# Attention inputs with a place each, V sums on two engines, softmax sums from a column of ones, logits by token

## The reference

```python
# q, k, v: [2, 8, 768, 64]; block, window = 32, 16
k_sum = k.reshape(B, H, nb, block, D).max(axis=3)
v_sum = v.reshape(B, H, nb, block, D).mean(axis=3)
scores_l = scale * q @ k.T, masked to |i - j| < window
scores_s = scale * q @ k_sum.T + log(block)
a = exp(concat(scores_l, scores_s) - max)
a = a / (sum(a) + 1e-09)
x = a @ concat(v, v_sum)                       # -> [1536, 512]
logits1 = x @ w_gate;  noise_scale = log1p(exp(x @ w_noise))
x1 = top-2 mixture of 8 experts (512 -> 1024 -> 512) of x
logits2 = x1 @ w_gate2;  skip = x1 @ w_skip
out = x1 + gate * chosen expert(x1) where skip > 0
```

## Time and profile before

| | us |
|---|---|
| median of 3 runs (lowest, highest) | 775.97 (775.58, 776.98) |
| the profiled execution's own time | 778.27 |
| its span, first to last instruction | 776.4 |
| PE busy (share of the span) | 667.5 (86%) |
| DVE / ACT / POOL busy | 378.0 / 322.7 / 201.1 |
| mean granted clock of PE | 0.948 |

### The profile page before, as it was taken

One profiled execution on the slowest core, in us unless ns is written; L12 is line 12 of the kernel. 1 busy time (PEld: TensorE's weight loads), 2 busy tenths in 40 slices (PEclk: granted clock), 3 DMA queues, 4 the chain that ended last, 5 costly groups with the idle time before them and its releaser, 6 DMA issues.

```text
span 776.4 us, 13848 instructions
## 1 busy us (share of the span) xinstructions
PE 667.5 (86%) x3906; PEld 534.9 (69%) x3906; DVE 378.0 (49%) x664; ACT 322.7 (42%) x613; POOL 201.1 (26%) x254
## 2 busy tenths in 40 slices
PE   4685876659999999999999999977569997999894
PEld 3464654448787887878878787855448776778673
DVE  3392685935453625434344345431636756556621
ACT  2272786025353524435244244422115656455511
POOL 1537330712222222232222222220221221222221
PEclk9996999779999999999999999997779999999998
DMA  9994795324555545635446264645326657667211
GB/s 204 193 210 134 205 279 188 129 82 135 149 160 150 151 94 138 161 70 156 117 118 183 48 176 125 173 118 182 148 82 189 191 173 261 205 196 230 55 39 16
DMA packets 91199, 116.67 MB, mean 150 GB/s; under 512 B 52500, under 2 KB 52500, under 8 KB 91088
## 3 DMA queue, kind: packets, MB, share of 16 engines
q1 hardware_dynamic: 81584, 94.75, 41.2%
q0 software_dynamic: 9568, 21.37, 14.7%
HBM read 99.72 MB, written 20.71 MB: 155 GB/s over the span
## 4 chain that ended last, share of the span: by engine, by line
PE 77%; DVE 6%; DMA 5%; issue 3%; POOL 3%; SPq 2%; ACT 2%; POOLq 0%; ACTq 0%; DVEq 0%
PE bank L690 60%; PE bank L706 5%; PE bank L616 3%; PE bank L665 3%; SPq L425 2%; DVE col_val L1168 2%; POOL stage L922 2%; DMA stage<-in_moe_w 2%; DMA stage<-in_v 1%; PE bank L605 1%; PE bank L577 1%; PE bank L767 1%; PE bank L588 1%; ACT pt_sb L800 1%; DVE w_lo L1077 1%
## 5 line engine op out<-in xcount | busy, mean ns | idle before, releaser
L1077 DVE TENSOR_TENSOR w_lo<-stage,w_hi (+1 forms) x128 | 152.0, 1221 | 29.6 <-ACT w_hi L807 27.5
L690 PE MATMUL bank<-w_hi,xt_hi 128*128 128x512 f32 x336 | 139.7, 416 | 16.3 <-DVE w_lo L1077 7.9
L1224 DVE TENSOR_TENSOR ht_lo<-bank,ht_hi 128x512 fp32r<-128x512 f32 x84 | 58.1, 691 | 185.2 <-ACT ht_hi L879 185.2
L807 ACT CAST w_hi<-stage (+1 forms) x128 | 129.1, 1049 | 28.2 <-PEq L732 23.6
L690 PE MATMUL bank<-w_hi,ht_hi 128*128 128x512 f32 x336 | 138.6, 412 | 0.0
L690 PE MATMUL bank<-w_lo,xt_hi 128*128 128x512 f32 x336 | 134.6, 401 | 0.0
L690 PE MATMUL bank<-w_lo,ht_hi 128*128 128x512 f32 x336 | 131.4, 391 | 0.0
L876 ACT ACTIVATE h_sb<-bank 128x512 f32<-128x512 f32 x84 | 50.3, 598 | 112.8 <-PE bank L690 112.8
L690 PE MATMUL bank<-w_hi,xt_lo 128*128 128x512 f32 x336 | 93.1, 400 | 0.0
L879 ACT CAST ht_hi<-bank 128x512 fp32r<-128x512 f32 x84 | 49.2, 586 | 100.9 <-PE bank L706 100.9
L690 PE MATMUL bank<-w_hi,ht_lo 128*128 128x512 f32 x336 | 91.1, 392 | 0.0
(11 more groups left out here) (111 smaller groups left out, 732.2 us busy)
## 6 DMA issues: line engine op xcount, KB each, us to landing
stage<-in_moe_w SPq DMA_DIRECT2D x128, 512.0 KB, 4.3
v_win<-in_v SPq DMA_DIRECT2D x24, 192.0 KB, 4.8
x_moe<-zeros SPq DMA_DIRECT2D x13, 256.0 KB, 4.3
stage<-in_k SPq DMA_DIRECT2D x16, 192.0 KB, 4.6
stage<-in_q SPq DMA_DIRECT2D x16, 192.0 KB, 4.4
stage<-in_v SPq DMA_DIRECT2D x16, 192.0 KB, 4.4
x_att<-x_sb SPq DMA_DIRECT2D x12, 256.0 KB, 4.1
x_sb<-x_moe SPq DMA_DIRECT2D x12, 256.0 KB, 2.8
```

The lines of the kernel that those rows point to most:

```text
L690: last = eng.matmul(ps[:], *every[i], start=(i == 0), stop=(i == len(every) - 1))
L807: eng.copy(piece(w_hi[n % SETS], j), stage[:, j, :]).then_inc(s_hi, 1)
L1077: eng.tensor_tensor(piece(w_lo[n % SETS], j), stage[:, j, :], piece(w_hi[n % SETS], j).bitcast(F32), ALU.subtract)\
L1224: eng.tensor_tensor(ht_lo[:, half].rearrange("p k n -> p (k n)"), ps_ht[half][:], ht_hi[:, half].bitcast(F32).rearrange("p k n -> p (k n)" ...
```

## The change

1. Places. K and Q of batch 0 and half of its V lie side by side in `stage`; the other half, and all of batch 1, in `late_raw`, which lies where the first expert's rounded weights (`w_hi0`, `w_lo0`) are written later. No load of K, Q or V waits any more. K and Q come by pairs of token tiles for all heads (256 KB a DMA), V by pairs of heads (384 KB a DMA). The constants are split: the identity first, the rest after the first Q.
2. Order. Q is turned two tiles at a time, when its tiles need it (steps 3 and 5); batch 1 follows in steps 6 to 12, V of batch 1 in step 13.
3. V is summed for heads 0 to 3 on POOL as before, for heads 4 to 7 by one reduction on DVE (line 1032 of the changed kernel).
4. `v_win` has a 65th column of ones for each head; the product with V gives the row sums in PSUM, `normalise` reads them there, and the exponentials have no accumulator. A head takes 74 columns in two joined banks.
5. Logits by token: the turned x is the stationary operand and `wgate` the moving one, straight into `ps_gate`. The copy on ACT and the transpose back are gone in both routers.
6. The first expert's pieces are loaded in tiles 2 to 5; the 13 blocks of zeros follow after the last store of x.

```diff
@@ -315,32 +329,30 @@
         STEPS = NG * NT
         TURN_LAG, PV_LAG = 2, 3
         NORM_LAG = NG - 1 + PV_LAG
-        X_LAG, GATE_LAG = NORM_LAG + 1, NORM_LAG + 2
-        LAST = STEPS - NG + GATE_LAG + 1
+        X_LAG, GATE_LAG = NORM_LAG + 1, NORM_LAG + 3
+        LAST = STEPS - NG + GATE_LAG
 
         def tile_at(s, lag):
...
-        late = [j for u in units[6:10] for j in unit_jobs(*u)]
+        def half_jobs(kind, b, j=0):
+            return [(kind, b, hh, j) for hh in range(2)]
+
+
+        at_step = {-1: [j for jj in range(JOBS) for j in half_jobs("k", 0, jj)] + half_jobs("q", 0, 0),
+                   2: half_jobs("v", 0), 3: half_jobs("q", 0, 1), 5: half_jobs("q", 0, 2),
+                   13: half_jobs("v", 1)}
+        late = [j for kind in "kq" for jj in range(JOBS) for j in half_jobs(kind, 1, jj)]
         for i, j in enumerate(late):
-            at_step.setdefault(2 + i * 8 // len(late), []).append(j)
-        for u, s in zip(units[10:], (10, 11)):
-            at_step.setdefault(s, []).extend(unit_jobs(*u))
-        UNITS0 = 9
-        UNITS_AT = {1: (9, 10), 2: (11,)}
-        VALUE_SUMS = {0: (4, 5), 7: (10,), 8: (11,)}
+            at_step.setdefault(6 + (i + 1) // 2, []).append(j)
+
+        POOL_SUMS = {0: (0, 0), 12: (1, 0)}
+        DVE_SUMS = {1: (0, 1), 11: (1, 1)}
         for s in range(LAST + 1):
...
-
-                if units[u][0] == "v":
-                    eng.wait_ge(s_vp, sum(x[0] == "v" for x in units[:u + 1]))
-                else:
-                    eng.wait_ge(s_tr, job_at[unit_jobs(*units[u])[-1]] + 1)
-
-            def load_unit(u):
-                kind, b, hh = units[u]
-                if u >= RR:
-                    wait_used(u - RR)
-                for i in range(UH):
-                    dst = by_head(u)[:, i] if kind == "v" else by_token(u)[:, :, i]
-                    src = {"k": k, "q": q, "v": v}[kind][b, hh * UH + i]
-                    rows = (src.rearrange("(p j) d -> p j d", j=VTOK) if kind == "v"
-                            else src.rearrange("(j p) d -> p j d", j=TOK))
-                    eng.dma_start(dst, rows).then_inc(s_raw[u % RR], 16)
...
             def load_piece(g):
 
                 n, j = divmod(g, PIECES)
-                if n == 0 and j // UP < RR:
-                    wait_used(len(units) - 1 - (len(units) - 1 - j // UP) % RR)
-                if n:
+                if n == 0:
+                    eng.wait_ge(s_tr, job_at["q", 0, 1, JOBS - 1] + 1)
+                    eng.wait_ge(s_vp[0], 1)
+                else:
...
+                for w in (2 * j - 2, 2 * j - 1):
+                    load_window(w)
+                load_tiles("q", 0, j)
+            for j in range(JOBS):
+                load_tiles("k", 1, j)
+            for w in range(4, WR):
                 load_window(w)
-            load_unit(6)
-            for w in range(2, 4):
-                load_window(w)
-            load_unit(7)
+            for j in range(JOBS):
+                load_tiles("q", 1, j)
+            for hh in range(2):
+                load_values(1, hh)
             eng.dma_start(wgate1[:, :, 0:E], m1_gate.rearrange("(k p) e -> p k e", p=P))\
                .then_inc(s_router, 16)
             eng.dma_start(wgate1[:, :, E:2 * E], m1_noise_w.rearrange("(k p) e -> p k e", p=P))\
...
-            for u in range(8, UNITS0):
-                load_unit(u)
-            eng.wait_ge(s_cast, 3)
             for t in range(NT):
-                for i in range((N // P + 1) * t // NT, (N // P + 1) * (t + 1) // NT):
-                    eng.dma_start(x1_dram[i * P:(i + 1) * P, :], zeros[:]).then_inc(s_zero, 16)
                 for w in (2 * t + WR, 2 * t + WR + 1):
                     if w < BATCH * NWIN:
                         load_window(w)
-                for u in UNITS_AT.get(t, ()):
-                    load_unit(u)
                 land(0)
-                if PIECE_TILE <= t < PIECE_TILE + PIECES // UP:
-                    for g in range(UP * (t - PIECE_TILE), UP * (t - PIECE_TILE + 1)):
+                if PIECE_TILE <= t < PIECE_TILE + PIECES // 2:
+                    for g in range(2 * (t - PIECE_TILE), 2 * (t - PIECE_TILE + 1)):
                         load_piece(g)
                 eng.wait_ge(s_x, t + 1)
                 eng.dma_start(x_dram[t * P:(t + 1) * P, :], x_sb[:, t % 2]).then_inc(s_xst[t % 2], 16)
+            land(0)
+            eng.wait_ge(s_cast, 3)
+            for i in range(N // P + 1):
+                eng.dma_start(x1_dram[i * P:(i + 1) * P, :], zeros[:]).then_inc(s_zero, 16)
             AIR = 4
             ready = (E + SETS) * PIECES
...
+                    eng.wait_ge(s_const, 16)
+                    eng.wait_ge(s_vp[job[2]], job[1] + 1)
                 else:
                     kind, b, hh, j = job
...
                                           start=True, stop=True)
                 last.then_inc(s_pv, 1)
 
             def router_logits(m, t, wgate, cols):
 
-
-                if t >= 2:
-                    eng.wait_ge(s_gte[m], t - 1)
+                if m == 0:
+
+                    eng.wait_ge(s_x, min(t + 2, NT))
                 for i in range(DK):
-                    last = eng.matmul(gt_place(m, t)[0:cols], wgate[:, i, 0:cols], xt2[t % 2][:, i, :],
-                                      start=(i == 0), stop=(i == DK - 1))
+                    last = eng.matmul(ps_gate[:, t * cols:(t + 1) * cols], xt2[t % 2][:, i, :],
+                                      wgate[:, i, 0:cols], start=(i == 0), stop=(i == DK - 1),
+                                      skip_group_check=True)
                 last.then_inc(s_gt[m], 1)
-
-            def turn_logits(m, t, cols):
-
-                eng.wait_ge(s_gte[m], t + 1)
-                eng.transpose(ps_gate[:, t * cols:(t + 1) * cols], gt_sb[0:cols, t % 2, :],
-                              ident[0:cols, 0:cols]).then_inc(s_gl[m], 1)
 
...
@@ -768,11 +759,9 @@
                                              x1_sb[:, t % XR, i * P:(i + 1) * P],
                                              ident)
                     last.then_inc(s_x1t, 1)
-                if 1 <= t <= NT:
+                if t:
                     eng.wait_ge(s_x1te[(t - 1) % 2], (t - 1) // 2 + 1)
                     router_logits(1, t - 1, wgate2, E + 1)
-                if t >= 2:
-                    turn_logits(1, t - 2, E + 1)
             ranks(1)
             lists(1)
             mixture(1)
...
                         empty_job(eng, job, eng.copy)
-                if (t := tile_at(s, GATE_LAG)) is not None:
-                    empty_gt(eng, 0, t, 2 * E)
+                if s == FIRST_SPLIT:
+
+                    eng.wait_ge(s_tr, job_at["q", 1, 1, JOBS - 1] + 1)
+                    for i in range(2):
+                        eng.wait_ge(s_vp[i], BATCH)
                 if 0 <= s - FIRST_SPLIT < PIECES:
                     round_piece(0, s - FIRST_SPLIT)
 
 
-            eng.wait_ge(s_gl[0], NT)
...
             AHEAD = 3
             for w in range(AHEAD):
                 window_of_keys(w)
             for w in range(BATCH * NWIN):
                 b = w // NWIN
-                for u in VALUE_SUMS.get(w, ()):
-                    value_sums(u)
+                if w in POOL_SUMS:
...
@@ -1040,6 +1024,14 @@
                                   keys.rearrange("p a (n s) -> p a n s", s=BLOCK),
                                   AX.X, ALU.max).then_inc(s_ksum, 1)
 
+            def value_sum(b, hh):
+
+                eng.wait_ge(s_rawv[b, hh], 16 * UH // 2)
+                if b:
+                    eng.wait_ge(s_tr, job_at["v", b - 1, hh, 0] + 1)
+                eng.tensor_reduce(v_part[hh][:], by_head(b, hh).rearrange("p h j d -> p h d j"),
+                                  AX.X, ALU.add).then_inc(s_vp[hh], 1)
+
             def softmax(s):
...
             def normalise(t):
-                eng.wait_ge(s_exp, GH * NG * (t + 1))
+                eng.wait_ge(s_pv, NG * (t + 1))
                 if t:
                     eng.wait_ge(s_x, t)
-                eng.tensor_scalar(rden[:], rsum[:, t % PR, :], EPS, None, ALU.add).then_inc(s_den, 1)
+                eng.tensor_scalar(rden[:], ps_heads[:, :, HD], EPS, None, ALU.add).then_inc(s_den, 1)
                 eng.wait_ge(s_den, 2 * t + 1)
                 eng.reciprocal(rden[:], rden[:]).then_inc(s_den, 1)
                 eng.wait_ge(s_den, 2 * t + 2)
-                eng.wait_ge(s_pv, NG * (t + 1))
                 if t >= 2:
                     eng.wait_ge(s_xst[t % 2], 16 * (t // 2))
                     eng.wait_ge(s_tr, job_at[("x", t - 2)] + 1)
                 eng.tensor_tensor(x_sb[:, t % 2].rearrange("p (h d) -> p h d", h=HEADS),
-                                  ps_x[:].rearrange("p (h d) -> p h d", h=HEADS),
+                                  ps_heads[:, :, 0:HD],
                                   rden[:].rearrange("p (h o) -> p h o", o=1)
```

164 lines of the change are left out of this document (83 added, 81 removed).

## The result

The changed kernel takes 781.39 us (median of 5 runs, 780.50 to 781.81), the kernel before 775.97 (774.73 to 778.51): a ratio of 1.0064, 95% interval 1.0043 to 1.0085. It is about 5 us slower, 0.6% and clear of the interval, where I had forecast 752.7 and a gain of 23.3. The profiled execution took 781.3 us, its span 779.5, 3.1 more than the span of before, whose profiled execution stood 2.3 above its median.

What follows compares the result with a forecast made beforehand. PE, 77% of the chain, was taken as the bound, with attention waiting on V and the first expert's pieces. Gains of 18.0 (attention), 0.3 (first router) and 5.0 (second router) sum to 23.3 us: 752.7 us, range 744 to 763.

Steps and rivals of the forecast that it cites:

- Logits by token, +5.0 us: Second router's loop: dropping the transpose back and swapping operands gains 0.38 us a tile, 5.0 us in all, bounds 0 and 8.
- the clock for longer: Rival in the attention: the wait near 55 us keeps PE at 1.2 GHz longer, about 761 us; chance 0.12.
- products above 0.97 us a tile: Sign of being wrong: the second router's loop would spend over 0.97 us a tile on products; 0.75 was forecast.
- Early start, 8 to 10 us gained and lost by tile 2: Attention start: tile 0 near 37 us instead of 44.50, but tile 2 at about 58, where it came at 57.48.
- the second of my two candidates: Attention: PE waits at step 7 for the router's small loads, near 55.5 us, with tile 4's scores behind it.
- The store, my first candidate: Attention: tile 0's store, queued on SP behind batch 1's loads, lands at about 58 us and holds tile 2's `normalise`.
- Tiles 3 and 4 at 6.5 us: Attention: with inputs on chip and two jobs of batch 1 each step, tiles 3 and 4 take 6.5 us each.
- Tiles 5 to 9: Attention: tile 5 takes 5.4 us, tiles 6 to 9 5.8 each; the last two tiles 4.6 and 4.9.
- the clock 1.5 us once: Attention: one stretch at 1.2 GHz after PE's wait near 50 to 58 us, costing 0 to 5, taken as 1.5.
- Half the clock beyond 70 us: Sign of being wrong: PE still at half its clock in the attention after 70 us.
- What was counted as nothing: Exponentials without the accumulator, 1.5 us of ACT at most, and zeros moved after tile 11, done by 127 us: neither counted.
- The chance of 0.04 for slower: Rival: the load stream runs at about 145 GB/s in place of 220, draining near 76 us: 776 to 780; chance 0.04.

Runs made afterwards that it cites:

- The kernel with POOL's sums: Changed kernel with router's small loads and stores of x on ACT's queue, and both halves of batch 1's V summed by POOL: 771.83 us, ratio 0.9939.
- their own run: Changed kernel with ACT's accumulation of the row sums put back beside the column of ones, written and not read: 778.28 us, ratio 1.0035.

## Why the prediction was wrong

**Logits by token, +5.0 us: the sign was wrong, and it decides the result.** The working had the operations right. A tile of 1.34 us was forecast and 1.28 is what it takes at the full clock. What failed is that I took the clock of the earlier trace rows for granted: those rows stand at 1.00 because the loop of before, which also starts at 1.2 GHz, brings the clock back some 4 us in, and the change took out of that loop the very products that do so. The edit taken back, the edit alone, and the four products or transposes added to each tile show it. I had weighed the weight loads at this place and not asked what the clock does there; "the clock for longer" was a rival of mine in the attention only. With it the loop costs 12 x 2.45 = 29.4 us and not 12 x 1.34 = 16.1, where it took 22.7 before. My own sign of being wrong, products above 0.97 us a tile, came: 1.57 from start to start (531.01 to 532.58).

**Early start, 8 to 10 us gained and lost by tile 2: right.** Tile 0 came at 37.73 (forecast 37). That it is this close is partly luck: in the traces of six kernels with the same attention it comes between 35.79 and 38.70. Tile 2 comes between 61.22 and 63.20 in all of them. The stream ended near 58: the store of tile 0 landed at 58.9 in one kernel, the last window at 59.4 in another.

**What holds tile 2: the second of my two candidates, and dearer.** I gave the router's five loads 3.0 us from the earlier trace rows, where they had been issued into a queue with room. Behind the full stream they took 7.3. PE's wait for them ended at 55.71, as forecast, but with the clock at 0.50 behind it tile 2 came at 61.91 in place of 58. That is 3.9 us; taking the wait away saved 3.0 in the trace and nothing in the median. The store, my first candidate, was issued at 54.91, landed at 58.7 and held nothing.

**Tiles 3 and 4 at 6.5 us: the step that failed in the attention.** They took 10.25 and 8.95, 6.2 us more than forecast. I took the pace of tiles 1 and 2 before. Of the 10.25, 1.5 is the clock (the stretch from 69 to 71.5): in four of the six kernels with the same attention tile 3 follows tile 2 at 8.74 or 8.75, in the others at 8.89 and 10.24, and with every load and window in time it is still 8.75. In these 8.75 us DVE has what it had from tile 0 to 1 before, three block maxima of 0.68 us and two copies of K, which took 6.77; new are the copy of x for the router and the 1.10 us in which DVE waits for scores that PE starts late. The forecast of 6.5 gave neither a price. DVE is nearly full (9.01 of 10 us), but which part costs what was not tested. DVE's reduction of V falls on tile 4, 3.75 us where I had 2.3 (and, as a bound, twice that), and I had priced it only in batch 0, behind POOL. The kernel with POOL's sums gives 1.6 us of this back from tile 3 to 4; why its median falls by 5.7 these two traces can't settle.

**Tiles 5 to 9: 3.0 us slower than forecast, the last two 0.65 faster.** The last of the three windows at 1.2 GHz falls on tile 9, which takes 6.97 us here and 5.81 in traces without that stretch; tile 5 took 6.72 in place of 5.4. I had given the clock 1.5 us once. Added up: 3.9 + 6.2 + 3.0 - 0.65 = 12.4 us, which is tile 11 at 121.66 in place of 109.2. "Half the clock beyond 70 us" was another of my signs, and it came twice.

**What was counted as nothing was nothing**: the exponentials by their own run, and the zeros by the trace, where POOL's first gather is issued at 154.31 without a wait for them. It follows tile 11 by 32.65 us in place of 31.5, since the last logits now run at 1.2 GHz (PEclk 0.56 from 122 to 127 us).

The chance of 0.04 for slower hung on one mechanism, a slow stream. The mechanism that came stood in none of my cases. What stays open: what it is in the loop by token that lets the clock fall about 10 us in even when PE comes to it at the full clock, and why the kernel with 56 or 78 transposes ahead of it differs by over 10 us from run to run. Products of widths between 9 and 128 columns were not tried.

## What to carry to other kernels

Before a product's operands are swapped or narrowed in a loop that PE sets, ask what brings PE to its full clock there, and price the loop at either clock: here 1.28 or 2.45 us a tile. When loads lose their waits, whatever stands behind them in the same queue, small loads and stores that hold a buffer above all, comes at the end of the stream; give those another queue or an earlier place. Idle work that keeps the clock up belongs behind the last signal that another engine waits for: ahead of it, 62 transposes held a gather up by 2 us and 84 products by 14; behind it the median fell by 4.3 us, a gain that the intervals don't quite separate from none.

## What the runs showed of the hardware

- Products of 9 streamed columns, with transposes between them, kept PE busy for 29.9 us at 1.2 GHz. In one run that came to them at 2.4 GHz the clock fell 9.9 us in, with PE busy throughout. Four products of 128 columns added to each tile brought 2.4 GHz back about 6.5 and 11 us in; four transposes of 128 columns did not in 39 us.
- Transposes alone, 6.9 us of them behind the lists, kept PEclk at 1.00 until the expert began, and the time (758.50 us) can't be told from that with products (757.21).
- A reduction on DVE of 2048 elements read at a pitch of 256 bytes took 3.67 to 3.78 us, 1.8 ns an element, where one of 512 neighbours took 0.68, 1.3 ns an element.
- Behind the stream SP took 0.45 and 0.54 us to issue the first two of the five small loads and 1.71, 2.12 and 2.31 for the others; before, the five took 3.0 together. The store of tile 0 landed 9.3 us after its issue from SP's queue behind the stream, and 4.9 us after its issue from ACT's queue beside it.
